# The end of an attention-and-two-MLPs kernel: turned row order in the last down parts, last sums in halves, one PSUM bank per output token row

## The chip, the cores and the metric

The kernel runs on one core of a Trainium2 chip. The metric is the device time of one execution in microseconds (us), as the median of several runs. Inputs and outputs are float32 in device memory.

## The reference

```python
def _attn_ref(x, weight_gen):            # x (2, 4096, 192), weight_gen (2, 4096, 8, 7)
    w = np.exp(weight_gen - np.max(weight_gen, axis=-1, keepdims=True))
    w = w / (np.sum(w, axis=-1, keepdims=True) + 1e-09)
    x_pad = np.concatenate([np.zeros((B, 6, D)), x], axis=1)
    x_unf = x_pad[:, np.arange(S)[:, None] + np.arange(7)[None, :], :].reshape(B, S, 7, 8, 24)
    return np.einsum('bshk,bskhg->bshg', w, x_unf).reshape(B, S, D)

def _moe_ref(x, w_in, w_out):            # w_in (192, 2048), w_out (2048, 192)
    h = x @ w_in
    return np.maximum(0.01 * h, h) @ w_out

def _moe2_ref(x, w_in, w_out):
    h = x @ w_in
    return np.where(h > 0.0, h, np.exp(np.minimum(h, 0.0)) - 1.0) @ w_out
```

The result is the second MLP of the first MLP of the attention's output, for 8192 tokens of 192 features.

## The kernel before, in words

**Tiling.** The 8192 tokens are cut into 16 chunks (CH) of 512 tokens (T): 128 partitions by 4 token rows (J). GpSimd and VectorE mix the seven taps of a chunk; then the chunk is turned so that features lie on partitions, and each MLP works on it in that form. The 192 features are carried as 128 ("a") and 64 ("b"). Products are made in split precision: a float32 operand is rounded into a "hi" part and a "lo" part, and hi times hi, lo times hi and hi times lo are added up in PSUM.

**Phases and steps.** A phase is one MLP on one chunk; there are 32 (0 to LAST = 31). Each has 8 steps (ST), numbered through as g = 0 to 255 (END). A step has an up part, which fills the 1024 columns of one half of the PSUM tensor `hidden`, an activation (ScalarE, VectorE), the rounding to `hid_hi` and the rest `hid_lo` (VectorE), and a down part of 20 matmuls, called by its step number d, which adds to the PSUM banks `y_a` (128 output features, 12 matmuls, helper `down_a`, L652) and `y_b` (64 features of the hi and the lo weights side by side on 128 partitions, 8 matmuls, helper `down_b`, L640). The down part of step d stands in TensorE's program beside the up part of step d + 3 (LAG). So the last three, d = 253, 254 and 255, have no up part beside them: they are the lone down parts (`down_alone` twice, `down_last` once).

**Row halves.** Every down matmul reads only 64 of the 128 rows of the hidden activations, LOW (partitions 0 to 63) or HIGH (64 to 127). A LOW and a HIGH matmul run side by side in the array, so 20 matmuls take ten places. Two matmuls of different halves that add to the same bank are kept apart by semaphores. In `y_b` all LOW matmuls of a part come first, then, behind a wait for `s_yblow`, all HIGH ones; the next part starts with LOW again, behind a wait for `s_dn`, which the part before raises with its last HIGH matmul. From d = 252 (APART) on `y_a` is summed apart, LOW in one bank and HIGH in the other, so that only `y_b` needs waits.

```python
                if d:
                    pe.wait_ge(s_dn, d)
                down_b(m, s, d, LOW, 0, 0)
```

**The last step.** Step 255 is made in halves of 512 columns on ScalarE and VectorE, and `down_last` waits for the first half of `hid_lo` (`s_lo1`), then for the second (`s_lo`).

**After the last matmul.** ScalarE copies one half of `y_a` into `ya` as soon as its matmuls are done (`s_yalast`, L925), and after the last matmul the 64 upper partitions of `y_b` into `ylow` (L919). VectorE then adds `yb` = `y_b` + `ylow` (L1129) and `ya` = `y_a` + `ya` (L1134), both for 512 columns. TensorE waits for both and turns the sums back to tokens (`transpose_last`): for each of the four token rows a 128x128 transpose of `ya` (L785) and a 64x64 one of `yb` (L786), two token rows to a bank of `hidden`. ScalarE copies the first two rows to `staged` (L940), VectorE the other two (L1251), and SyncE stores each half of `staged` with a DMA of its own (L499) when its copy is done. The end of the program waits for these DMAs.

Each engine runs its own program in the order written; the order is written out by hand in the functions below.

## Time and profile before

| | |
|---|---|
| median of 3 runs | 1143.02 us (1142.68 to 1144.25) |
| the profiled execution, its time | 1143.43 us |
| its span, first to last instruction | 1141.4 us |
| mean granted TensorE clock | 0.996 |
| TensorE matmul busy | 1126.3 us, 99% of the span |
| ScalarE, VectorE, GpSimd busy | 741.3 us (65%), 628.0 us (55%), 392.1 us (34%) |
| chain that ended last, share of TensorE | 97% |

TensorE is busy nearly the whole span; the rows used below come from its last 17 us, and a few from its first 60 us where the same kinds of instruction run. A matmul's row gives its start and a modelled length, and two rows of different halves can have the same start. "Before" in the notes in square brackets at a row's end is idle time of the engine and what ended it.

### The profile page before, as it was taken

The numbers are of one execution on the slowest core, as the hardware profiler recorded it, in microseconds if no ns is written. First come the engines' busy times: TensorE is split into PE (matmuls) and PEld (weight loads), VectorE is DVE, ScalarE is ACT, GpSimd is POOL, SyncE is SP. The second block draws the span as 40 slices with busy tenths as digits, with TensorE's granted clock in tenths as the row PEclk, the third lists the DMA queues.
The fourth block names the chain that finished last, engine by engine and source line by source line (L and its number), as shares of the span: only waits on it lengthen the run. The fifth ranks groups of instructions, "written<-read, shape, count | busy, mean of one in ns | idle before, by whom it ended". The sixth has DMA issues, their size and how long they took to land.

```text
span 1141.4 us, 22701 instructions
## 1 busy us (share of the span) xinstructions
PE 1126.3 (99%) x9804; PEld 923.7 (81%) x9804; DVE 628.0 (55%) x659; ACT 741.3 (65%) x830; POOL 392.1 (34%) x409
## 2 busy tenths in 40 slices
PE   6999999999999999999999999999999999999998
PEld 4778888888888888888888888888888888888886
DVE  7857737456464554636456464554736546364554
ACT  3666757567575765757667576665757667575774
POOL 5835340805317071350804308062260804400000
PEclk9999999999999999999999999999999999999999
DMA  5313021020202102021020211202021020110001
GB/s 178 107 63 95 1 81 29 29 82 1 90 20 69 41 29 81 1 81 29 29 81 1 81 29 44 67 15 84 12 81 29 29 81 2 43 29 29 15 1 56
DMA packets 44723, 55.45 MB, mean 49 GB/s; under 512 B 4116, under 2 KB 32914, under 8 KB 44624
## 3 DMA queue, kind: packets, MB, share of 16 engines
q1 hardware_dynamic: 44624, 54.01, 15.4%
q8 instruction: 77, 1.26, 0.5%
q14 instruction: 22, 0.18, 0.1%
HBM read 36.29 MB, written 17.69 MB: 47 GB/s over the span
## 4 chain that ended last, share of the span: by engine, by line
PE 97%; POOL 1%; DVE 1%; ACT 1%; DMA 1%; issue 0%; SPq 0%; POOLq 0%; ACTq 0%
PE y_a L652 31%; PE hidden L553 30%; PE y_b L640 20%; PE hidden L557 10%; PE hidden L608 5%; DMA xw<-in_x_dram 1%; DVE hid_lo L1178 0%; POOL prod L345 0%; ACT hid_hi L967 0%; POOL act L348 0%; POOL staged L345 0%; POOL act L345 0%; PE hidden L609 0%; PE hidden L785 0%; DVE dn L377 0%
## 5 line engine op out<-in xcount | busy, mean ns | idle before, releaser
L652 PE MATMUL y_a<-hid_hi,dn 64*128 64x512 f32 x2048 | 626.9, 386 | 0.1
L652 PEld LDWEIGHTS y_a<-hid_hi,dn 64*128 64x128 f32 x2048 | 375.8, 184 | 40.9 <-PE y_a L652 1.0
L640 PE MATMUL y_b<-hid_hi,dn 64*128 64x512 f32 x1024 | 396.1, 387 | 0.5 <-PE y_b L640 0.2
L640 PE MATMUL y_b<-hid_lo,dn 64*128 64x512 f32 x1024 | 395.4, 386 | 0.0
L652 PE MATMUL y_a<-hid_lo,dn 64*128 64x512 f32 x1024 | 394.6, 386 | 0.0
L1178 DVE TENSOR_TENSOR hid_lo<-hidden,hid_hi 128x1024 fp32r<-128x1024 f32 x128 | 156.5, 1223 | 256.8 <-ACT hid_hi L967 256.6
L553 PE MATMUL hidden<-in_a_hi,up_a_hi 64*128 64x512 f32 x1020 | 295.5, 388 | 2.2 <-DVE hid_lo L1178 1.7
L553 PE MATMUL hidden<-in_a_lo,up_a_hi 64*128 64x512 f32 x1020 | 294.7, 386 | 0.0
L553 PE MATMUL hidden<-in_a_hi,up_a_lo 64*128 64x512 f32 x1020 | 294.7, 386 | 0.0
L557 PE MATMUL hidden<-in_b,up_b_hi 64*128 64x512 f32 x1020 | 294.7, 386 | 0.0
L1178 DVE TENSOR_TENSOR hid_lo<-act,hid_hi 128x1024 fp32r<-128x1024 f32 x127 | 158.9, 1251 | 190.3 <-ACT hid_hi L967 190.3
L949 ACT ACTIVATE hidden<-hidden 128x1024 f32<-128x1024 f32 x127 | 128.0, 1008 | 199.3 <-PE hidden L557 199.3
L951 ACT ACTIVATE act<-hidden 128x1024 f32<-128x1024 f32 x127 | 130.5, 1027 | 160.9 <-PE hidden L557 159.1
L321 POOL TENSOR_TENSOR mix<-xw,wk 128x384 f32<-128x384 f32 x30 | 26.4, 880 | 573.9 <-DVE wk L1097 568.5
L640 PEld LDWEIGHTS y_b<-hid_hi,dn 64*128 64x128 f32 x1024 | 188.4, 184 | 21.9 <-issue 2.0
L652 PEld LDWEIGHTS y_a<-hid_lo,dn 64*128 64x128 f32 x1024 | 188.4, 184 | 20.0
L640 PEld LDWEIGHTS y_b<-hid_lo,dn 64*128 64x128 f32 x1024 | 188.4, 184 | 19.8
L333 POOL TENSOR_TENSOR mix<-mix,prod 128x384 f32<-128x384 f32 x180 | 191.9, 1066 | 2.4
L1153 DVE SCALAR_TENSOR_TENSOR act<-act,hidden 128x1024 f32<-128x1024 f32 x129 | 155.7, 1207 | 45.6 <-ACT act L956 45.1
L321 POOL TENSOR_TENSOR prod<-xw,wk 128x384 f32<-128x384 f32 x180 | 169.5, 949 | 9.4
L553 PEld LDWEIGHTS hidden<-in_a_hi,up_a_hi 64*128 64x128 f32 x1020 | 140.9, 184 | 25.3 <-issue 2.1
L553 PEld LDWEIGHTS hidden<-in_a_lo,up_a_hi 64*128 64x128 f32 x1020 | 141.0, 184 | 20.0
(109 smaller groups left out, 1318.8 us busy)
## 6 DMA issues: line engine op xcount, KB each, us to landing
xw<-in_x_dram SPq DMA_DIRECT2D x14, 960.0 KB
raw_b<-squares_out SPq DMA_DIRECT2D x60, 96.0 KB, 2.2
out_dram<-staged SPq DMA_DIRECT2D x15, 384.0 KB, 2.6
squares_in<-prod SPq DMA_DIRECT2D x56, 96.0 KB, 2.0
squares_out<-ya SPq DMA_DIRECT2D x15, 256.0 KB, 2.0
raw_a<-squares_in SPq DMA_DIRECT2D x14, 256.0 KB, 2.9
raw_d<-in_moe_w_out_dram SPq DMA_DIRECT2D x8, 384.0 KB, 3.4
raw_a<-in_moe_w_in_dram SPq DMA_DIRECT2D x8, 256.0 KB, 3.5
```

What stands on the lines that cost most here:

```text
L321: ops.tensor_tensor(dst, src, w, ALU.mult).then_inc(done, 1)
L333: ops.tensor_tensor(mix[:, j0:j1, :], mix[:, j0:j1, :], terms[k % n][:, j0:j1, :], ALU.add).then_inc(done, 1)
L553: return nc.tensor.matmul(hidden[:, s % 2, HALF[i]], w[m][rows, cols], v[src][rows, :], start=start, stop=stop)
L557: return nc.tensor.matmul(hidden[:, s % 2, HALF[i]], up_b_hi[m][rows, cols], in_b[src][rows, :], start=False, stop=stop)
L608: low = nc.tensor.matmul(hidden[:, s % 2, HALF[0]], up_b_lo[m][LOW, cols], in_b[src][LOW, :], start=False, stop=stop)
L640: return nc.tensor.matmul(y_b[d // ST % 2][:, :], dn[m][rows, f, P:2 * P], v[rows, s % HB, HALF[i]], start=start, stop=stop)
L652: return nc.tensor.matmul(y_a[bank][:, :], dn[m][rows, f, w:w + P], v[rows, s % HB, HALF[i]], start=start, stop=stop)
L949: nc.scalar.activation(hidden[:, s % 2, :], hidden[:, s % 2, :], ACT.Prelu, alpha=SLOPE).then_inc(s_leak, 1)
L951: nc.scalar.activation(act[:, s % 2, :], hidden[:, s % 2, :], ACT.Relu, scale=-1.0).then_inc(s_relu, 1)
L1153: nc.vector.scalar_tensor_tensor(out=a, in0=a, scalar=-1.0, in1=h, op0=ALU.add, op1=ALU.max).then_inc(done, 1)
L1178: nc.vector.tensor_tensor(hid_lo[:, s % HB, :], (act if m else hidden)[:, s % 2, :], hid_hi[:, s % HB, :].bitcast(f32), ALU.subtract).then ...
```

## The change

Three things are changed, all behind the last up part.

1. **The lone down parts.** Part 253 (new function `down_reversed`) and part 255 (`down_last`, rewritten) run the row halves the other way round: `y_b` HIGH first, then behind a wait LOW; part 254 stays as it was. So 252 ends with `y_b` HIGH and 253 begins with it, 253 ends with LOW and 254 begins with it, and so on; the wait for `s_dn` in front of 253, 254 and 255 is gone. `s_yblow` is called `s_ybfirst`. The half of `y_a` that is ready early is now LOW. `down_last` waits for the second half of `hid_lo` behind its fifth matmul, not its sixth.
2. **The last sums.** New function `add_last`: VectorE waits for the last matmul itself, adds `ya` first, in two halves of 256 columns (two token rows each), then `yb` in two halves. It no longer waits for `ylow` ahead of `ya`.
3. **The transposes.** Each token row goes to a bank of its own. Order: `ya` rows 0 and 1, `yb` rows 0 and 1, `ya` rows 2 and 3, `yb` rows 2 and 3, each group behind a wait for its half of the sum. ScalarE copies rows 0 and 2 to `staged`, VectorE rows 1 and 3; each of the two last stores waits for both engines.

TensorE's program, part 254's end and part 255 up to the sixth matmul, before (the name in front of the arrow is the PSUM bank written; L640 is `down_b`, L652 `down_a`):

```order
L652 MATMUL y_a0<-hid_lo,dn1 128x512
L640 MATMUL y_b1<-hid_lo,dn1 128x512
L640 MATMUL y_b1<-hid_hi,dn1 128x512 [waits down_done,half_hidden_lo_ready]
L652 MATMUL y_a1<-hid_hi,dn1 128x512
L640 MATMUL y_b1<-hid_lo,dn1 128x512
L652 MATMUL y_a1<-hid_hi,dn1 128x512
L652 MATMUL y_a0<-hid_hi,dn1 128x512
L652 MATMUL y_a1<-hid_lo,dn1 128x512
L640 MATMUL y_b1<-hid_hi,dn1 128x512 [waits hidden_lo_ready]
```

and the same place now (L642 is `down_b`, L654 `down_a`):

```order
L654 MATMUL y_a0<-hid_lo,dn1 128x512
L642 MATMUL y_b1<-hid_lo,dn1 128x512
L654 MATMUL y_a0<-hid_hi,dn1 128x512 [waits half_hidden_lo_ready]
L642 MATMUL y_b1<-hid_hi,dn1 128x512
L654 MATMUL y_a0<-hid_hi,dn1 128x512
L642 MATMUL y_b1<-hid_lo,dn1 128x512
L654 MATMUL y_a0<-hid_lo,dn1 128x512
L642 MATMUL y_b1<-hid_hi,dn1 128x512 [waits hidden_lo_ready]
L654 MATMUL y_a0<-hid_hi,dn1 128x512
```

The wait for the part before (down_done) is gone, and the wait for the second half of `hid_lo` has moved one matmul forward.

TensorE's transposes, before:

```order
L785 MATMUL hidden<-ident,ya 128x128 [waits y_b_added,y_a_copied]
L786 MATMUL hidden<-ident,yb1 128x64
L785 MATMUL hidden<-ident,ya 128x128
L786 MATMUL hidden<-ident,yb1 128x64
L785 MATMUL hidden<-ident,ya 128x128
L786 MATMUL hidden<-ident,yb1 128x64
L785 MATMUL hidden<-ident,ya 128x128
L786 MATMUL hidden<-ident,yb1 128x64
```

and now:

```order
L810 MATMUL hidden<-ident,ya 128x128 [waits y_a_copied]
L810 MATMUL hidden<-ident,ya 128x128
L813 MATMUL hidden<-ident,yb1 128x64 [waits y_b_added]
L813 MATMUL hidden<-ident,yb1 128x64
L810 MATMUL hidden<-ident,ya 128x128 [waits y_a_copied]
L810 MATMUL hidden<-ident,ya 128x128
L813 MATMUL hidden<-ident,yb1 128x64 [waits y_b_added]
L813 MATMUL hidden<-ident,yb1 128x64
```

The eight transposes are the same; they stand in pairs of one kind, with four waits in place of one.

VectorE's last four instructions before the end, before (L1129, L1134 and L1251 and the one ahead):

```order
L1167 TENSOR_TENSOR hid_lo<-act,hid_hi 128x512 [waits hidden_hi_ready]
L1129 TENSOR_TENSOR yb1<-y_b1,ylow 64x4x4x32 [waits squares_out_written,y_low_copied]
L1134 TENSOR_TENSOR ya<-y_a0,ya 128x4x4x32 [waits y_a_high_rows_copied]
L1251 COPY staged<-hidden 128x384 [waits out_stored,out_transposed]
L68 UNCONDITIONAL_BRANCH
```

and now:

```order
L1208 TENSOR_TENSOR hid_lo<-act,hid_hi 128x512 [waits hidden_hi_ready]
L1170 TENSOR_TENSOR ya<-y_a1,ya 128x4x2x32 [waits y_a_high_rows_copied,down_done]
L1170 TENSOR_TENSOR ya<-y_a1,ya 128x4x2x32
L1175 TENSOR_TENSOR yb1<-y_b1,ylow 64x4x2x32 [waits squares_out_written,y_low_copied]
L1175 TENSOR_TENSOR yb1<-y_b1,ylow 64x4x2x32
L1293 COPY staged<-hidden 128x192 [waits out_transposed,out_stored]
L1293 COPY staged<-hidden 128x192 [waits out_transposed]
```

Two adds have become four and one copy has become two; ScalarE's one copy (L940) has become two of 192 columns as well (L973).

The diff, cut to its core:

```diff
-        out_turn = hidden[:, 0, :]
+        out_bank = [hidden[:, j // 2, j % 2 * T:j % 2 * T + D] for j in range(J)]
...
+        BEHIND_REVERSED = (END - 1,)
...
-            for i, done, count in ((0, s_stag, CH), (1, s_stagv, 1)):
-                sp.wait_ge(done, count)
+            for i in (0, 1):
+                sp.wait_ge(s_stag, CH + i)
+                sp.wait_ge(s_stagv, 1 + i)
...
-                if d:
+                if d and d not in BEHIND_REVERSED:
...
+            def down_reversed(m, s, d):
+                pe.wait_ge(s_lo, d + 1)
+                down_a(m, s, d, LOW, 0, 0)
+                down_b(m, s, d, HIGH, 0, 0)
+                down_a(m, s, d, LOW, 0, 1)
+                down_b(m, s, d, HIGH, 0, 1)
+                down_a(m, s, d, LOW, 0, 2)
+                down_b(m, s, d, HIGH, 1, 0)
+                down_a(m, s, d, LOW, 1, 0)
+                down_b(m, s, d, HIGH, 1, 1).then_inc(s_ybfirst, 1)
+                if d < ST:
+                    pe.wait_ge(s_dn, d)
+                down_a(m, s, d, LOW, 1, 1)
+                down_a(m, s, d, HIGH, 0, 0)
+                down_a(m, s, d, LOW, 1, 2)
+                down_a(m, s, d, HIGH, 0, 1)
+                pe.wait_ge(s_ybfirst, d + 1)
+                down_b(m, s, d, LOW, 0, 0)
+                down_a(m, s, d, HIGH, 0, 2)
+                down_b(m, s, d, LOW, 0, 1)
+                down_a(m, s, d, HIGH, 1, 0)
+                down_b(m, s, d, LOW, 1, 0)
+                down_a(m, s, d, HIGH, 1, 1)
+                down_b(m, s, d, LOW, 1, 1)
+                down_a(m, s, d, HIGH, 1, 2).then_inc(s_dn, 1)
...
             def transpose_last():
...
+                for h in (0, 1):
+                    pe.wait_ge(s_ya, CH + h)
+                    turn_a(2 * h)
+                    turn_a(2 * h + 1)
+                    pe.wait_ge(s_yb, LAST + 1 + h)
+                    turn_b(2 * h)
+                    turn_b(2 * h + 1)
...
-            for d in range(LAG - 1, 0, -1):
-                down_alone(1, ST - 1 - d, END - d)
+            down_reversed(1, ST - 3, END - 2)
+            down_alone(1, ST - 2, END - 1)
             down_last()
...
-                nc.scalar.activation(staged[:, 0, :], out_turn[:, 0:2 * D], ACT.Copy).then_inc(s_stag, 1)
+                for j in (0, 2):
+                    act_e.wait_ge(s_outt, j + 1)
+                    nc.scalar.activation(staged[:, j // 2, 0:D], out_bank[j], ACT.Copy).then_inc(s_stag, 1)
...
+            def add_last():
+                dve.wait_ge(s_dn, END + 1)
+                dve.wait_ge(s_ya1, 1)
+                a, a0 = last_columns(ya[:, :], True), last_columns(y_a[LAST % 2][:, :], False)
+                b, b0, b1 = last_columns(yb[1][:, :], True), last_columns(y_b[LAST % 2][0:D2, :], False), last_columns(ylow[:, :], False)
+                halves = slice(0, J // 2), slice(J // 2, J)
+                for js in halves:
+                    nc.vector.tensor_tensor(a[:, :, js], a0[:, :, js], a[:, :, js], ALU.add).then_inc(s_ya, 1)
+                dve.wait_ge(s_ylow, LAST + 1)
+                dve.wait_ge(s_outw, 32 * (CH - 1))
+                for js in halves:
+                    nc.vector.tensor_tensor(b[:, :, js], b0[:, :, js], b1[:, :, js], ALU.add).then_inc(s_yb, 1)
...
-            nc.vector.tensor_copy(staged[:, 1, :], out_turn[:, T:T + 2 * D]).then_inc(s_stagv, 1)
+            for j in (1, 3):
+                dve.wait_ge(s_outt, j + 1)
+                nc.vector.tensor_copy(staged[:, j // 2, D:2 * D], out_bank[j]).then_inc(s_stagv, 1)
```

## Rows read from the trace of the kernel before

**Rows 1.** The page: the chain that ended last, by engine.

```profile
PE 97%; POOL 1%; DVE 1%; ACT 1%; DMA 1%; issue 0%; SPq 0%; POOLq 0%; ACTq 0%
```

**Rows 2.** The timeline of TensorE: start us, length us, instruction; parts 252 and 253.

```profile
1124.92 0.39 PE L640 MATMUL y_b<-hid_hi,dn 64*128 64x512 f32 x1
1125.14 0.39 PE L640 MATMUL y_b<-hid_lo,dn 64*128 64x512 f32 x1
1125.68 0.47 PE L640 MATMUL y_b<-hid_hi,dn 64*128 64x512 f32 x1 [0.15 <-PE y_b L640]
1125.99 0.39 PE L640 MATMUL y_b<-hid_lo,dn 64*128 64x512 f32 x1
1126.22 0.39 PE L640 MATMUL y_b<-hid_hi,dn 64*128 64x512 f32 x1
...
1126.45 0.39 PE L640 MATMUL y_b<-hid_lo,dn 64*128 64x512 f32 x1
...
1127.18 0.39 PE L640 MATMUL y_b<-hid_hi,dn 64*128 64x512 f32 x1
...
1127.40 0.39 PE L640 MATMUL y_b<-hid_lo,dn 64*128 64x512 f32 x1
...
1127.86 0.39 PE L640 MATMUL y_b<-hid_lo,dn 64*128 64x512 f32 x1
```

**Rows 3.** The same view, parts 254 (first row) and 255.

```profile
1128.39 0.46 PE L640 MATMUL y_b<-hid_hi,dn 64*128 64x512 f32 x1
...
1131.12 0.47 PE L640 MATMUL y_b<-hid_hi,dn 64*128 64x512 f32 x1
...
1132.12 0.39 PE L640 MATMUL y_b<-hid_lo,dn 64*128 64x512 f32 x1
...
1132.60 0.47 PE L640 MATMUL y_b<-hid_hi,dn 64*128 64x512 f32 x1
...
1133.37 0.39 PE L640 MATMUL y_b<-hid_lo,dn 64*128 64x512 f32 x1
```

**Rows 4.** The timeline of VectorE: `hid_lo` of step 254, then of step 255 in halves.

```profile
1125.85 1.23 DVE L1178 TENSOR_TENSOR hid_lo<-act,hid_hi 128x1024 fp32r<-128x1024 f32 x1 [0.24 <-ACT hid_hi L967]
...
1128.75 1.47 DVE L1167 TENSOR_TENSOR hid_lo<-act,hid_hi 128x512 fp32r<-128x512 f32 x2
```

**Rows 5.** The timeline of all engines behind the last matmul.

```profile
1133.80 0.59 ACT L919 ACTIVATE ylow<-y_b 64x512 f32<-64x512 f32 x1 [0.41 <-PE y_b L640]
1134.43 0.68 DVE L1129 TENSOR_TENSOR yb<-y_b,ylow 64x512 f32<-64x512 f32 x1 [4.21 <-ACT ylow L919]
1135.04 0.67 DVE L1134 TENSOR_TENSOR ya<-y_a,ya 128x512 f32<-128x512 f32 x1
...
1135.76 0.35 PE L785 MATMUL hidden<-ident,ya 128*128 128x128 f32 x1 [2.00 <-DVE ya L1134]
...
1136.04 0.37 PE L786 MATMUL hidden<-ident,yb 64*128 64x64 f32 x1
...
1136.34 0.47 PE L785 MATMUL hidden<-ident,ya 128*128 128x128 f32 x1
...
1136.74 0.37 PE L786 MATMUL hidden<-ident,yb 64*128 64x64 f32 x1
...
1138.14 0.37 PE L786 MATMUL hidden<-ident,yb 64*128 64x64 f32 x1
1138.55 0.56 DVE L1251 COPY staged<-hidden 128x384 f32<-128x384 f32 x1 [2.84 <-PE hidden L786]
1139.13 0.33 SPq L499 DMA_DIRECT2D out_dram<-staged  x1
```

**Rows 6.** Busy time by stretch; the third number from the end is the granted clock.

```profile
1135.50:1135.70 0.20, 0.00 (x0) 0.00 (x0) 0.20 (x1) 0.00 (x0) 0.00 (x0) 1.00 0.00 0
1135.90:1136.00 0.10, 0.10 (x1) 0.00 (x0) 0.00 (x0) 0.00 (x0) 0.00 (x0) 0.69 0.00 0
1136.00:1136.10 0.10, 0.10 (x2) 0.06 (x1) 0.00 (x0) 0.00 (x0) 0.00 (x0) 0.50 0.00 0
```

**Rows 7.** The timeline near the start: 128x128 products at the lower and the higher clock, and a reader.

```profile
9.28 1.87 PE L760 MATMUL y_b<-ident,prod 128*128 128x128 f32 x8 [2.78 <-POOL prod L345]
...
19.54 1.09 PE L764 MATMUL y_a<-ident,act 128*64 128x128 f32 x8
...
20.67 0.59 ACT L891 ACTIVATE in_b_up<-y_a 64x512 fp32r<-64x512 f32 x1 [0.42 <-PE y_a L764]
```

**Rows 8.** The timeline at 52 us: VectorE on 256 columns, and its next start.

```profile
52.37 0.41 DVE L376 TENSOR_TENSOR dn<-raw_d,dn 128x256 fp32r<-128x256 f32 x1
...
52.70 0.69 DVE L377 TENSOR_TENSOR dn<-raw_d,dn 128x512 fp32r<-128x512 f32 x1
```

More of the change, by code:

```diff
@@ L638, in down_b @@
                 v = (hid_hi, hid_lo)[n]
-                start, stop = f == 0 and n == 0 and rows == LOW, f == FT - 1 and n == 1 and rows == HIGH
+                start, stop = f == 0 and n == 0 and rows == LOW, f == FT - 1 and n == 1 and rows == (LOW if d == END else HIGH)
                 return nc.tensor.matmul(y_b[d // ST % 2][:, :], dn[m][rows, f, P:2 * P], v[rows, s % HB, HALF[i]], start=start, stop=stop)
@@ L672, in down_open @@
                 down_a(m, s, d, HIGH, 0, 2)
-                down_b(m, s, d, LOW, 1, 1).then_inc(s_yblow, 1)
+                down_b(m, s, d, LOW, 1, 1).then_inc(s_ybfirst, 1)
                 down_a(m, s, d, HIGH, 1, 0)
@@ L720, in down_last @@
                 wait_half_end(pe, s_lo, s_lo1, 0)
[L721 removed]
+                down_a(1, s, d, LOW, 0, 0)
+                down_b(1, s, d, HIGH, 0, 0)
+                down_a(1, s, d, LOW, 0, 1)
+                down_b(1, s, d, HIGH, 0, 1)
+                down_a(1, s, d, LOW, 0, 2)
+                wait_half_end(pe, s_lo, s_lo1, 1)
+                down_b(1, s, d, HIGH, 1, 0)
+                down_a(1, s, d, LOW, 1, 0)
+                down_b(1, s, d, HIGH, 1, 1).then_inc(s_ybfirst, 1)
+                down_a(1, s, d, LOW, 1, 1)
+                down_a(1, s, d, HIGH, 0, 0)
+                down_a(1, s, d, LOW, 1, 2).then_inc(s_yalast, 1)
+                down_a(1, s, d, HIGH, 0, 1)
+                pe.wait_ge(s_ybfirst, END + 1)
                 down_b(1, s, d, LOW, 0, 0)
[L723 removed]
+                down_a(1, s, d, HIGH, 0, 2)
                 down_b(1, s, d, LOW, 0, 1)
[L725 to L729 removed]
+                down_a(1, s, d, HIGH, 1, 0)
                 down_b(1, s, d, LOW, 1, 0)
[L731 to L732 removed]
                 down_a(1, s, d, HIGH, 1, 1)
[L734 to L745 removed]
+                down_b(1, s, d, LOW, 1, 1)
+                down_a(1, s, d, HIGH, 1, 2).then_inc(s_dn, 1)
             def sum_first_mix():
@@ L778, in transpose_last, with turn_a, turn_b @@
             def transpose_last():
-                pe.wait_ge(s_ya, CH)
-                pe.wait_ge(s_yb, LAST + 1)
-                for j in range(J):
-                    o = (j % 2) * D
-                    o += (j // 2) * T
-                    nc.tensor.transpose(out_turn[:, o:o + P], ya[:, j * P:(j + 1) * P], ident[:, :])
-                    last = nc.tensor.transpose(out_turn[:, o + P:o + D], yb[1][:, j * P:(j + 1) * P], ident[0:D2, 0:D2])
-                    if j % 2:
-                        last.then_inc(s_outt, 1)
+                def turn_a(j):
+                    nc.tensor.transpose(out_bank[j][:, 0:P], ya[:, j * P:(j + 1) * P], ident[:, :])
+                def turn_b(j):
+                    nc.tensor.transpose(out_bank[j][:, P:D], yb[1][:, j * P:(j + 1) * P], ident[0:D2, 0:D2]).then_inc(s_outt, 1)
+                for h in (0, 1):
[5 more added lines that the diff above has]
+                    turn_b(2 * h + 1)
             def phase(m, c, ph, dm, dc):
@@ L924, in take_y @@
                     act_e.wait_ge(s_outw, 32 * dc)
[L925 removed]
+                    nc.scalar.activation(last_columns(ya[:, :], True), last_columns(y_a[1 - ph % 2][:, :], False), ACT.Copy).then_inc(s_ya1, 1)
                     copy_low()
@@ L1126, in add_y @@
                 dst, b0, b1 = yb[dm][:, :], y_b[ph % 2][0:D2, :], ylow[:, :]
-                if ph == LAST:
-                    dst, b0, b1 = last_columns(dst, True), last_columns(b0, False), last_columns(b1, False)
                 nc.vector.tensor_tensor(dst, b0, b1, ALU.add).then_inc(s_yb, 1)
-                if ph == LAST:
-                    dve.wait_ge(s_ya1, 1)
-                    whole = last_columns(ya[:, :], True)
-                    nc.vector.tensor_tensor(whole, last_columns(y_a[1 - ph % 2][:, :], False), whole, ALU.add).then_inc(s_ya, 1)
+            def add_last():
[10 more added lines that the diff above has]
+                    nc.vector.tensor_tensor(b[:, :, js], b0[:, :, js], b1[:, :, js], ALU.add).then_inc(s_yb, 1)
             def turn_mix(c):
```

28 lines of the change are left out of this document (3 added, 25 removed).

## The prediction

> **What bounds the kernel now.** I read the page's chain first: 97% of the chain that ended last is TensorE [rows 1]. So a microsecond counts only where TensorE stands still or where nothing of it is left, and the change touches nothing ahead of the last up part. I therefore read only the last 17 us: the timeline of TensorE over the lone down parts, VectorE's timeline over the same stretch, then all engines behind the last matmul.
>
> The reader is to see three things. First, in steady state the pairs of a down part start 0.227 us apart, but between part 252 and 253 they start at 1125.14, 1125.68, 1125.99 and 1126.22 [rows 2]: three places take 1.08 us in place of 0.68, so the wait for the part before costs 0.40. The same gap, 0.53 and 0.54 from start to start, stands ahead of 254 (1127.86 to 1128.39) and of 255 [rows 2, 3]. Second, inside part 255 the last LOW matmul of `y_b` starts at 1132.12 and the first HIGH one at 1132.60 with a long first row, 0.47 [rows 3]: there too the drain shows. Third, from the start of the last matmul, 1133.37, to the issue of the last store, 1139.13, 5.76 us pass in single file: 0.43 to ScalarE's copy, its 0.59, two adds of 0.68 and 0.67 that start 0.61 apart, eight transposes from 1135.76 to 1138.14, a copy of 0.56 [rows 3, 5]. After the issue come 2.27 us to the span's end at 1141.4.
>
> **The lone parts.** The last pair of 252 starts at 1125.14 and the last of 255 at 1133.37: 8.23 us for 30 places. At 0.227 each they would take 6.81. All of the 1.42 goes if no wait is felt. Three boundaries are 1.20 of it, part 255's middle wait and small slips the rest. Do new waits take their place? The turned parts keep a wait in the middle, for the fourth `y_b` HIGH matmul, but now the first LOW one stands three places later, 0.68 us; a dependent matmul started 0.54 after its forerunner [rows 2], so it fits. Behind that wait stand all further matmuls of both halves, so if it did not fit, each part would pay up to the 0.40 of a boundary. `hid_lo` is the next thing that can be late. Part 254 would start at 1127.64 and its `hid_lo` ends at 1127.08; part 255 at 1129.91, its first half being ready near 1129.45. The second half is done at 1130.22 [rows 4], and TensorE now wants it ahead of the third pair, 1130.36, with the weight load in front of that. I charge 0.10 (bounds 0 and 0.40). ScalarE's and VectorE's work there does not wait for these down parts, so they get no earlier and no later. Gain 1.32; last pair at 1132.05.
>
> **The sums.** ScalarE's early copy of `y_a` starts 0.43 behind the sixth place of 255 and is done near 1132.1, ahead of need. VectorE can start 0.43 behind the last pair, at 1132.48. What half an add costs the tail does not show. Upper bound: as much as a whole one, 0.61 from start to start; lower: half of that. The nearest row has 256 columns: 0.41 long, the next starting 0.33 later [rows 8]. I take it. `ya` halves start at 1132.48 and 1132.81, `yb` halves at 1133.14 and 1133.47, ended at 1133.55 and 1133.88; `ylow` is ready at 1133.07 (0.59 behind 1132.48) and hides behind the `ya` adds. Were those faster, `ylow` would set the pace. Splitting is what a rule speaks against. The Trainium skill (Perfetto Trace Analysis, section "Optimizing Scalar/DVE Operations") gives VectorE an overhead of about 125 ns for each instruction that reads PSUM, and advises larger operations where the engine is saturated. As an estimate from that page the two extra adds cost 0.25, where the row's spacing implies 0.07 above 256 columns at the rate of the long rows, and the sum would be 0.1 worse by it.
>
> **The transposes.** A transpose starts 0.05 behind the add it waits for [rows 5]. Before, each change of kind costs a place of 0.40 (from `ya` to `yb`) or 0.30 (back), at a granted clock of 0.50; the first, mostly at full clock, took 0.28 [rows 5, 6]. Products of one kind in a row took 0.14 at the higher clock and 0.23 at the lower (1.09 and 1.87 for eight) [rows 7]. The granted clock fell from 1.00 to 0.50 (2.4 to 1.2 GHz) at about 1135.93, behind a stretch from 1133.76 in which TensorE did nothing but the first transpose [rows 6], 2.17 us after the last matmul ended. Now the standstill before the first transpose is 0.5 us, and all are through 2.4 us after the last matmul's end. I take the higher clock. First `ya` at 1132.94, second 1133.08; first `yb` at 1133.60 (1133.55 and 0.05), then 1133.74, `ya` 1134.02 and 1134.16, `yb` 1134.44 and 1134.58. A change of kind counts 0.28 (bounds 0.14 and 0.40). Its last row is 0.27 long (0.37, less 0.10 for the clock, as 0.47 became 0.35), and a reader starts 0.04 behind such a row (1138.51 to 1138.55; 20.63 to 20.67) [rows 5, 7]: 1134.89.
>
> **Copies and stores.** VectorE's copy of 384 columns took 0.56; 192 fewer at 1.09 ns, from 0.67 for 512 and 1.23 for 1024 [rows 4, 5], leave 0.35, bounds 0.28 and 0.56. It ends at 1135.24, the store is issued at 1135.26. ScalarE's row 2 copy runs beside. The first store now waits for both engines, but has both near 1134.4, and its issue is over before the second's; it costs nothing. If the two transfers met, the second would be later by at most its own 0.6 us of data. The bank of its own costs nothing: it lets two engines read while TensorE writes.
>
> **Sum.** From the last pair to the issue 3.21 us in place of 5.76: 2.55. With 1.32 the gain is 3.87: the profiled execution of 1143.43 would be 1139.56. It stands 0.41 above the median, which I keep: 1143.02 less 3.87 is **1139.2 us**. A measurement of this kernel can tell about 0.2%, 2.29 us, from no change; that bound is 1140.7.
>
> **Rivals.** (A) The clock falls before or during the new transposes. For: it did in the same place before. Against: the standstill is a quarter as long. Places of 0.23, 0.30 and 0.40 and a last row of 0.37 put the issue at 1135.77: gain 3.36, **1139.7**. The Trainium skill (TensorE: Matmul & The Clock Gate, section "Part 4: PE-mode transpose") says that transposes do not count as work for the clock; by that rule the eight would be part of the standstill and A likelier. The trace fits it as far as it goes: the clock fell while a transpose ran. (B) Halves cost as much as wholes. The last `yb` half ends at 1134.99 and the copy takes 0.56: gain 3.06, **1140.0**. For: short instructions near 0.4 us carry a large fixed part. Against: rows 8. (C) The drain in the middle of the two turned parts is felt, 0.40 each, so TensorE gains 0.52: gain 3.07, **1140.0**. Against: 0.68 is above 0.54, and in part 253 before, with the same distance, the wait cost nothing: 1126.45 to 1127.18 is three places and 0.05 [rows 2]. (D) A, B and C together: gain 2.07, **1141.0**, within 0.2%. (E) The other side: the turned parts lose their pairing. Their matmuls begin with `y_a` LOW beside `y_b` HIGH, an order that only the end of a part had. If each half waited for the other, 20 pairs would take 0.227 more each, 4.54: **1143.7**, slower than before; from 17 lost pairs on the gain is eaten, and on top of D it would be 1145.5. Against: the closing pairs of every part are just this mixture and run at 0.23 (1127.18, 1127.40) [rows 2].
>
> **How the numbers follow.** Forecast 0.50, A 0.20, B 0.08, C 0.10, D 0.08, E 0.04 (half of it within 0.2%, half slower). Faster by over 0.2%: 0.50 + 0.20 + 0.08 + 0.10 = 0.88. Within: 0.08 + 0.02 = 0.10. Slower: 0.02. Range: upward to D, 1141.1. Downward the cheap bounds: no wait for `hid_lo` (0.10), a change of kind at 0.14 (0.28), a copy of 0.28 (0.07), and some 0.3 by which runs of one kernel differ: 1138.4.
>
> **What would show it.** TensorE's last down pair should start near 1132.05 with no gap of 0.54 at 253, 254 and 255; VectorE's `ya` half some 0.43 behind it; spacing 0.33 of the adds; granted clock 1.00 through the transposes and the last of them near 1134.6; the last store issued near 1135.3. A gap at the seventh place of 253 or 255 would be C, a clock of 0.50 A, adds of 0.6 B, rows of one half alone E. If the span shrinks by less than 2 us though all this holds, the tail behind the last store has grown, and the sum misses it.

## The result and the profile after

The changed kernel took 1138.93 us, median of 7 runs (1138.55 to 1139.19), beside 1142.75 us for the kernel before on the same chip (median of 7, 1142.67 to 1144.25). The ratio is 0.9964, 95% interval 0.9953 to 0.9975: faster by 0.36%. Forecast: 1139.2, range 1138.4 to 1141.1.

| | before | after |
|---|---|---|
| the profiled execution, its time | 1143.43 us | 1139.19 us |
| its span | 1141.4 us | 1137.4 us |
| mean granted clock | 0.996 | 1.000 |
| TensorE matmul busy | 1126.3 us | 1125.1 us (99%) |
| ScalarE, VectorE, GpSimd busy | 741.3, 628.0, 392.1 us | 741.6, 628.4, 392.0 us |

The page of the changed kernel, the chain that ended last by engine, reads as [rows 1] did:

```profile
PE 97%; POOL 1%; DVE 1%; DMA 1%; ACT 0%; issue 0%; SPq 0%; POOLq 0%; ACTq 0%
```

TensorE's timeline in the changed kernel (start, length), the places that answer to [rows 2, 3]. L642 is now `down_b`, L654 `down_a`.

```profile
1125.22 0.39 PE L642 MATMUL y_b<-hid_lo,dn 64*128 64x512 f32 x1
...
1125.45 0.39 PE L642 MATMUL y_b<-hid_hi,dn 64*128 64x512 f32 x1
...
1126.13 0.39 PE L642 MATMUL y_b<-hid_lo,dn 64*128 64x512 f32 x1
...
1126.81 0.39 PE L642 MATMUL y_b<-hid_hi,dn 64*128 64x512 f32 x1
...
1127.49 0.39 PE L642 MATMUL y_b<-hid_lo,dn 64*128 64x512 f32 x1
...
1127.71 0.39 PE L642 MATMUL y_b<-hid_hi,dn 64*128 64x512 f32 x1
...
1130.44 0.42 PE L642 MATMUL y_b<-hid_hi,dn 64*128 64x512 f32 x1
...
1130.70 0.38 PE L642 MATMUL y_b<-hid_lo,dn 64*128 64x512 f32 x1
...
1132.08 0.39 PE L654 MATMUL y_a<-hid_lo,dn 64*128 64x512 f32 x1
```

The first two rows are the last pair of 252 and the first of 253: 0.23 apart, where 0.54 stood. From the fourth `y_b` HIGH (1126.13) to the first LOW (1126.81) it is 0.68, three places, and the LOW row has its normal length: the middle wait is not felt. 253 passes to 254 (1127.49, 1127.71) without a gap, and 254 to 255 too (1129.76, 1129.98, not shown). The row at 1130.44 is the one behind the wait for the second half of `hid_lo`, which was ready at 1130.31: 0.42 long, its follower 0.26 behind it, a slip of 0.03 to 0.04. From the last pair of 252 to the last of 255 it is 6.86 us (1125.22 to 1132.08), 8.23 before: 1.37 gained.

All engines behind the last matmul, answering to [rows 5]; "x2" is a group of two, whose length runs from the first's start to the second's end:

```profile
1131.54 0.60 ACT L958 ACTIVATE ya<-y_a 128x512 f32<-128x512 f32 x1 [1.96 <-PE y_a L654]
...
1132.50 0.59 ACT L952 ACTIVATE ylow<-y_b 64x512 f32<-64x512 f32 x1 [0.36 <-PE y_a L654]
1132.59 0.76 DVE L1170 TENSOR_TENSOR ya<-y_a,ya 128x256 f32<-128x256 f32 x2 [2.28 <-PE y_a L654]
...
1133.07 0.44 PE L810 MATMUL hidden<-ident,ya 128*128 128x128 f32 x2 [0.61 <-DVE ya L1170]
1133.26 0.74 DVE L1175 TENSOR_TENSOR yb<-y_b,ylow 64x256 f32<-64x256 f32 x2
...
1133.72 0.33 PE L813 MATMUL hidden<-ident,yb 64*128 64x64 f32 x2 [0.22 <-DVE yb L1175]
...
1133.99 0.44 PE L810 MATMUL hidden<-ident,ya 128*128 128x128 f32 x2
...
1134.36 0.33 PE L813 MATMUL hidden<-ident,yb 64*128 64x64 f32 x2
1134.60 0.90 SPq L501 DMA_DIRECT2D out_dram<-staged  x2
...
1134.73 0.36 DVE L1293 COPY staged<-hidden 128x192 f32<-128x192 f32 x1 [0.21 <-PE hidden L813]
```

Read it as two files of work that overlap. VectorE no longer waits for `ylow`: that copy and the `ya` adds start together. TensorE starts on the first half of `ya` while VectorE is on the next sum. From the start of the last down matmul to the end of VectorE's last copy it is 3.01 us (1132.08 to 1135.09), before 5.74 (1133.37 to 1139.11, [rows 3, 5]). Behind it 2.3 us remain to the span's end, as before.

Busy time by stretch (third number from the end: granted clock), over the last transposes and over the stores:

```profile
1134.20:1134.80 0.60, 0.49 (x4) 0.20 (x2) 0.39 (x2) 0.36 (x2) 0.00 (x0) 1.00 0.00 0
1135.00:1137.40 2.40, 0.00 (x0) 0.00 (x0) 0.09 (x1) 0.00 (x0) 0.00 (x0) 1.00 0.46 164
```

Where [rows 6] show the clock fall, here it stays at 1.00 to the end of the span, though TensorE does nothing in the second stretch. The account of the spans: 1.37 in the lone parts, 8.03 to 5.32 from the last down matmul's start to the span's end (2.71), less 0.08 by which part 252 ended later: 4.00.

### The profile page after: what moved, and what is told of

Read it like the earlier page. It is cut to its first block, busy times and chain, and to the rows that moved or that the text cites. A ratio compares the mean times of both kernels' runs of the same rounds, so it can differ in the third digit from the quotient of the medians.

```text
span 1137.4 us, 22704 instructions
## 1 busy us (share of the span) xinstructions
PE 1125.1 (99%) x9804; PEld 923.7 (81%) x9804; DVE 628.4 (55%) x662; ACT 741.6 (65%) x831; POOL 392.0 (34%) x409
## 4 chain that ended last, share of the span: by engine, by line
PE 97%; POOL 1%; DVE 1%; DMA 1%; ACT 0%; issue 0%; SPq 0%; POOLq 0%; ACTq 0%
PE y_a L654 31%; PE hidden L555 30%; PE y_b L642 20%; PE hidden L559 10%; PE hidden L610 5%; DMA xw<-in_x_dram 1%; DVE hid_lo L1219 0%; POOL prod L346 0%; ACT hid_hi L1000 0%; POOL act L349 0%; POOL staged L346 0%; POOL act L346 0%; PE hidden L611 0%; DVE dn L378 0%; PE y_b L789 0%
## 5 line engine op out<-in xcount | busy, mean ns | idle before, releaser
L654 PE MATMUL y_a<-hid_hi,dn 64*128 64x512 f32 x2048 | 626.6, 386 | 0.1
L654 PEld LDWEIGHTS y_a<-hid_hi,dn 64*128 64x128 f32 x2048 | 375.9, 184 | 41.0 <-PE y_a L654 1.0
L642 PE MATMUL y_b<-hid_hi,dn 64*128 64x512 f32 x1024 | 395.8, 386 | 0.0
L642 PE MATMUL y_b<-hid_lo,dn 64*128 64x512 f32 x1024 | 395.3, 386 | 0.0
L654 PE MATMUL y_a<-hid_lo,dn 64*128 64x512 f32 x1024 | 394.7, 386 | 0.0
L642 PEld LDWEIGHTS y_b<-hid_hi,dn 64*128 64x128 f32 x1024 | 188.4, 184 | 20.3 <-issue 0.4
L654 PEld LDWEIGHTS y_a<-hid_lo,dn 64*128 64x128 f32 x1024 | 188.4, 184 | 20.2
L642 PEld LDWEIGHTS y_b<-hid_lo,dn 64*128 64x128 f32 x1024 | 188.4, 184 | 20.0
L559 PEld LDWEIGHTS hidden<-in_b,up_b_hi 64*128 64x128 f32 x1020 | 141.0, 184 | 20.0
```

The costliest lines, as they stand in the source:

```text
L559: return nc.tensor.matmul(hidden[:, s % 2, HALF[i]], up_b_hi[m][rows, cols], in_b[src][rows, :], start=False, stop=stop)
L642: return nc.tensor.matmul(y_b[d // ST % 2][:, :], dn[m][rows, f, P:2 * P], v[rows, s % HB, HALF[i]], start=start, stop=stop)
L654: return nc.tensor.matmul(y_a[bank][:, :], dn[m][rows, f, w:w + P], v[rows, s % HB, HALF[i]], start=start, stop=stop)
```

## The experiments

Ratios are to the kernel before on the same chip, with the 95% interval. The variants ran on other chips than the first comparison; the kernel before took 1142.47, 1142.85 and 1142.90 us there (medians), so compare ratios, not times, across rows. One comparison is independent of the start of the run: from the last pair of part 252 (a `y_b` row of `hid_lo`) to that of 255 ("lone parts"), and from there to the end of VectorE's last copy ("tail"). It is needed because the first product of the mix (`ident`, `prod`, near the start) begins anywhere from 8.88 to 10.54 us in these profiles, and all behind it moves along.

| kernel | time, us | ratio | lone parts | tail | span |
|---|---|---|---|---|---|
| before | 1142.75 | | 8.23 | 5.74 | 1141.4 |
| before again | 1142.32 (one) | | 8.23 | 4.90 | 1140.2 |
| changed | 1138.93 | 0.9964 [0.9953, 0.9975] | 6.86 | 3.01 | 1137.4 |
| changed again | 1139.05 (one) | | 6.86 | 3.01 | 1137.3 |
| changed, parts as before | 1140.14 | 0.998 [0.9971, 0.9989] | 8.22 | 3.03 | 1139.8 |
| before, parts turned | 1141.4 | 0.999 [0.9981, 0.9999] | 6.86 | 5.70 | 1139.9 |
| whole sums | 1139.24 | 0.9971 [0.996, 0.9982] | 6.87 | 3.20 | 1137.3 |
| copies of two rows | 1139.11 | 0.9969 [0.9957, 0.998] | 6.85 | 3.29 | 1137.4 |
| kinds alternating | 1139.54 | 0.9972 [0.9961, 0.9983] | 6.86 | 3.70 | 1137.8 |
| sums interleaved | 1138.83 | 0.9963 [0.9951, 0.9976] | 6.86 | 2.96 | 1137.0 |
| and `ylow` in halves | 1138.57 | 0.9962 [0.9948, 0.9976] | 6.87 | 2.74 | 1136.8 |
| nearer waits | 1139.15 (one) | | 7.30 | 3.07 | 1137.4 |

Most steps between the changed kernel and its variants are smaller than the intervals; there the profile's rows decide, not the times.

### One half of the change alone

The changed kernel with the lone parts as before:

```diff
-            down_reversed(1, ST - 3, END - 2)
-            down_alone(1, ST - 2, END - 1)
+            for d in range(LAG - 1, 0, -1):
+                down_alone(1, ST - 1 - d, END - d)
...
-                if d and d not in BEHIND_REVERSED:
+                if d:
```

and `down_last` in its old order.

> The changed kernel with its sums, transposes and copies, but with the three lone down parts in the old order and the waits for the part before in place. My account (two separate gains): TensorE's last down pair starts 1.3 to 1.4 us later than in the changed kernel, with gaps of 0.54 us ahead of 253, 254 and 255, and everything behind it stands as it did; span near 1138.8, 2.6 us below the kernel before (1141.4). Rival (one gain only: the shorter sums would be covered by something else, or the turning carries it all): span within 0.5 us of 1141.4 or of 1137.4.

Its TensorE timeline, from the last pair of 252:

```profile
1126.24 0.39 PE L641 MATMUL y_b<-hid_lo,dn 64*128 64x512 f32 x1
...
1126.78 0.47 PE L641 MATMUL y_b<-hid_hi,dn 64*128 64x512 f32 x1 [0.15 <-PE y_b L641]
...
1128.96 0.39 PE L641 MATMUL y_b<-hid_lo,dn 64*128 64x512 f32 x1
...
1129.49 0.47 PE L641 MATMUL y_b<-hid_hi,dn 64*128 64x512 f32 x1
```

The gaps of 0.54 and 0.53 and the long first rows are back, the tail is 3.03. Its lone parts are 8.22 (1126.24 to 1134.46). The span of 1139.8 overstates the loss: the first mix product started at 10.54 (9.29 in the changed kernel) and part 252 ended 1.02 later. Without that the loss is 1.4.

The other half, only the lone parts turned, in the kernel before (the same functions, the tail untouched).

> The kernel before with nothing but the three lone down parts turned. My account: the last down pair starts near 1132.1, and the 5.76 us from it to the issue of the last store stay, transposes at a granted clock of 0.50; span near 1140.0, 1.4 below the kernel before. With e1 the gains should add up to the whole 4.0. Rival: with the matmuls closer the transposes keep the higher clock and the gain is 2 us or more; or it is lost behind the last matmul and the span stays at 1141.4.

Lone parts 6.86, tail 5.70, the granted clock again at 0.50 from the second transpose on. So by the rows the two halves of the change don't interact: 1.37 by the one, about 2.7 by the other, at these clocks. The medians say 1.07 and 2.33; their intervals (0.1 to 2.2 and 1.3 to 3.3) hold the rows' numbers but are too wide to check the sum.

### The sums

Whole adds of 512 columns, still `ya` first and each row in its bank:

```diff
-                halves = slice(0, J // 2), slice(J // 2, J)
+                halves = (slice(0, J),)
```

> The changed kernel with each of the two last sums added whole (512 columns), 128-feature sum still first, transposes in the same order. My account: first yb transpose 0.2 to 0.3 us later than 1.64 behind the last down pair, all behind it later by the same; span 0.2 to 0.3 longer than the changed kernel (1137.4). Rival (halves pay their fixed part twice and give nothing): span equal to the changed kernel or shorter.

VectorE's adds and the first transpose that waits for `yb`:

```profile
1132.21 0.69 DVE L1170 TENSOR_TENSOR ya<-y_a,ya 128x512 f32<-128x512 f32 x1 [2.29 <-PE y_a L654]
1132.82 0.67 DVE L1175 TENSOR_TENSOR yb<-y_b,ylow 64x512 f32<-64x512 f32 x1
...
1133.55 0.33 PE L813 MATMUL hidden<-ident,yb 64*128 64x64 f32 x2
```

It starts 1.83 behind the last pair (1131.72), 1.64 in the changed kernel, and all behind it is 0.19 later. As for what a half costs: two of `ya` take 0.76 where the whole takes 0.69. The Trainium skill (Perfetto Trace Analysis, section "Optimizing Scalar/DVE Operations") puts an instruction's overhead at about 125 ns; the extra one cost 0.07 here, and the split pays. The same section also advises to break up instructions of an engine that isn't saturated but holds up others, which is this case; the prediction named only its advice against splitting.

Sums in the order `ya`, `yb`, `ya`, `yb`:

```diff
                 for js in halves:
                     nc.vector.tensor_tensor(a[:, :, js], a0[:, :, js], a[:, :, js], ALU.add).then_inc(s_ya, 1)
-                dve.wait_ge(s_ylow, LAST + 1)
-                dve.wait_ge(s_outw, 32 * (CH - 1))
-                for js in halves:
+                    dve.wait_ge(s_ylow, LAST + 1)
+                    dve.wait_ge(s_outw, 32 * (CH - 1))
                     nc.vector.tensor_tensor(b[:, :, js], b0[:, :, js], b1[:, :, js], ALU.add).then_inc(s_yb, 1)
```

> The changed kernel with the four half sums in the order ya, yb, ya, yb. My account: ylow is ready 1.01 us behind the last down pair, the first yb half then ends 1.46 behind it in place of 1.59, the first yb transpose starts 0.12 earlier and so does all behind it; span 1137.3. Rival (the wait for ylow stands in front of the second ya half and pushes the last yb half back): the last yb transpose starts no earlier or up to 0.1 later, span 1137.4 or more.

The first `yb` transpose came 0.12 earlier (1.52 behind the last pair), as expected, but the end only 0.05: VectorE now waits for `ylow` inside the file of sums (its second instruction starts 0.55 behind the first, not 0.34), so the second half of `ya` ends at 1133.48 and the second pair of its transposes can start only at 1133.53, 0.33 behind the first pair of `yb` in place of 0.27. The wait for `ylow` showed what to try next, `ylow` copied in halves too:

```diff
-                    copy_low()
+                    for js in (slice(0, J // 2), slice(J // 2, J)):
+                        nc.scalar.activation(low[:, :, js], low0[:, :, js], ACT.Copy).then_inc(s_ylow, 1)
...
-                    dve.wait_ge(s_ylow, LAST + 1)
+                    dve.wait_ge(s_ylow, LAST + (1 if js.start == 0 else 2))
```

> The order of e7 (ya, yb, ya, yb halves) and ScalarE's copy of the upper partitions of y_b in two halves of 256 columns as well. My account: ylow's first half is ready 0.77 us behind the last down pair in place of 1.01, the four adds run without a gap from 0.50 on at a spacing of 0.33, the first yb half ends at 1.25 and the second at 1.91; first yb transpose at 1.30 (changed kernel 1.64, e7 1.52), second pair at 1.96 (changed 2.28, e7 2.22), last copy ends at 2.70 (changed 3.01). Median about 0.3 us below the changed kernel's. Rival (the copy's halves pay their fixed part twice and the second yb half waits for ylow's second half): second pair of yb transposes at 2.2 or later, no gain over e7.

```profile
1131.72 0.39 PE L654 MATMUL y_a<-hid_lo,dn 64*128 64x512 f32 x1
1132.14 0.65 ACT L963 ACTIVATE ylow<-y_b 64x256 f32<-64x256 f32 x2 [0.37 <-PE y_a L654]
1132.22 0.42 DVE L1174 TENSOR_TENSOR ya<-y_a,ya 128x256 f32<-128x256 f32 x1 [2.29 <-PE y_a L654]
1132.56 0.41 DVE L1177 TENSOR_TENSOR yb<-y_b,ylow 64x256 f32<-64x256 f32 x1
...
1133.07 0.34 PE L813 MATMUL hidden<-ident,yb 64*128 64x64 f32 x2
...
1133.72 0.33 PE L813 MATMUL hidden<-ident,yb 64*128 64x64 f32 x2
```

The four halves follow each other at 0.34 again, and the tail is 2.74 where 2.70 was expected. This version has the shortest tail and the lowest median, 0.36 below the changed kernel's but on another chip. The ratios (0.9962 and 0.9964) don't separate the two; the 0.27 of the profile's rows is what is shown.

### The order of the transposes

`ya`, `yb`, `ya`, `yb` row by row, as before the change, with banks and halves as after it:

```diff
                     turn_a(2 * h)
-                    turn_a(2 * h + 1)
                     pe.wait_ge(s_yb, LAST + 1 + h)
                     turn_b(2 * h)
+                    turn_a(2 * h + 1)
                     turn_b(2 * h + 1)
```

> The changed kernel with the transposes in the old alternating order (ya, yb, ya, yb of rows 0 and 1, then of 2 and 3), each in its own bank. My account: at the higher clock a change of kind costs about 0.13 more than a place of the same kind, and one ya transpose can no longer hide ahead of the first yb; the last transpose starts 0.6 to 0.8 us later than in the changed kernel (1134.49), span near 1138.1. Rival (a change of kind costs nothing at the higher clock): last transpose 0.15 later, span near 1137.6.

```profile
1133.39 0.27 PE L813 MATMUL hidden<-ident,yb 64*128 64x64 f32 x1 [0.33 <-DVE yb L1175]
...
1133.59 0.33 PE L810 MATMUL hidden<-ident,ya 128*128 128x128 f32 x1
...
1133.85 0.27 PE L813 MATMUL hidden<-ident,yb 64*128 64x64 f32 x1
...
1134.05 0.33 PE L810 MATMUL hidden<-ident,ya 128*128 128x128 f32 x1
```

At full clock a change of kind costs a place of 0.20 (from `yb` to `ya`) or 0.26 (back). In the changed kernel a pair of one kind ends 0.33 (`yb`) or 0.44 (`ya`) behind its start, that is 0.06 and 0.11 more than one transpose alone (0.27, 0.33). From the end of the first `yb` transpose to the end of the last it is six changes of kind and 1.38 us here, two changes and 0.70 in the changed kernel; the tail is 0.69 longer. One of the six transposes in that stretch is a `ya` that the changed kernel has already done while it waits for `yb`, so the 0.69 is the price of the order, not of the changes of kind alone. The span grew by 0.4 only, because part 252 ended 0.34 earlier than in the changed kernel's profile. This is the largest single piece that an experiment took out of the tail.

### The copies

Two token rows to a bank again, one copy of 384 columns by each engine, each store behind one engine. Pairing and halves stay:

```diff
-                for j in (0, 2):
-                    act_e.wait_ge(s_outt, j + 1)
-                    nc.scalar.activation(staged[:, j // 2, 0:D], out_bank[j], ACT.Copy).then_inc(s_stag, 1)
+                act_e.wait_ge(s_outt, 2)
+                nc.scalar.activation(staged[:, 0, :], hidden[:, 0, 0:2 * D], ACT.Copy).then_inc(s_stag, 1)
```

and the same on VectorE.

> The changed kernel with two token rows to a bank again and one copy of 384 columns on each engine, each store behind its own engine. My account: VectorE's last copy 0.56 in place of 0.36 us, so the last store is issued 0.2 later and the span is 0.2 longer (1137.6); the first store is issued about as early as before. Rival (the two stores meet, so the last one's end is set by the first): with the first store's start unchanged the span stays at 1137.4.

```profile
1134.10 0.34 PE L812 MATMUL hidden<-ident,yb 64*128 64x64 f32 x2
1134.55 0.56 DVE L1290 COPY staged<-hidden 128x384 f32<-128x384 f32 x1 [0.80 <-PE hidden L812]
```

The last copy takes 0.56 in place of 0.36, and starts 0.45 behind the transposes in place of 0.37: tail 3.29, 0.28 more. The span stayed at 1137.4, the rival's number, but only because part 252 ended 0.25 earlier in this profile. From the copy's end to the span's end it is 2.29, 2.31 in the changed kernel, so the two last stores do not get in each other's way in either form.

### The clock

Three copies of 768 columns, whose results nobody reads, ahead of VectorE's first sum, so that TensorE stands still as long as in the kernel before:

```diff
+                for spot in (raw_d[:, 4:8, :], mix[:, :, :], prod2[:, :, :]):
+                    nc.vector.tensor_copy(spot, raw_d[:, 0:4, :])
                 for js in halves:
```

> The changed kernel with three copies of 768 columns on VectorE ahead of the last sums, whose results nobody reads, so that TensorE stands still for some 2 to 3 us more before the transposes. Account A (the higher clock of the changed kernel's transposes comes from the short standstill): the granted clock falls to 0.50 before or during the transposes, and the stretch from the first yb transpose to the last goes from 0.77 to 1.1 us or more. Rival (the clock was kept for another reason, such as the order in pairs): clock 1.00 and the stretch stays at 0.77.

```profile
1133.99 0.44 PE L810 MATMUL hidden<-ident,ya 128*128 128x128 f32 x2 [2.00 <-DVE ya L1172]
...
1134.64 0.34 PE L813 MATMUL hidden<-ident,yb 64*128 64x64 f32 x2 [0.22 <-DVE yb L1177]
...
1135.28 0.33 PE L813 MATMUL hidden<-ident,yb 64*128 64x64 f32 x2
```

The stretches around the last pair (third number from the end: granted clock):

```profile
1135.20:1135.40 0.20, 0.20 (x4) 0.13 (x2) 0.20 (x1) 0.14 (x1) 0.00 (x0) 1.00 0.00 0
1135.40:1135.60 0.20, 0.20 (x2) 0.07 (x2) 0.04 (x1) 0.01 (x1) 0.00 (x0) 0.76 0.00 0
```

The idle time ahead of the first transpose is 2.00, exactly that of [rows 5], and still the transposes ran at 1.00, but for the last 0.1 us of the last pair; its pairs of `yb` start 0.64 apart, as in the changed kernel. The fall came 3.5 us behind the end of the last down matmul, not 2.17. Time 1140.12 (one run).

The kernel before, unchanged, once more.

> The kernel before once more, for the clock at its transposes and for the time at which its first products start. If the fall differs from run to run, it comes again somewhere between 2.2 and 4.9 us behind the last down matmul, so part or all of the transposes, which run from 2.0 to 4.7 us behind it, are at 0.50; a fall later than in the first profile would shorten the stretch of the transposes (2.38 us) by up to 0.9. From the last down pair of part 252 to the last of 255 8.2 us again.

```profile
1135.44 0.33 PE L785 MATMUL hidden<-ident,ya 128*128 128x128 f32 x1 [2.00 <-DVE ya L1134]
...
1137.09 0.27 PE L786 MATMUL hidden<-ident,yb 64*128 64x64 f32 x1
1137.39 0.56 DVE L1251 COPY staged<-hidden 128x384 f32<-128x384 f32 x1 [2.01 <-PE hidden L786]
```

```profile
1137.10:1137.40 0.30, 0.26 (x2) 0.12 (x1) 0.01 (x1) 0.00 (x0) 0.00 (x0) 1.00 0.00 0
```

The same program, all eight transposes at full clock: 1.65 us from the first start to the last in place of 2.38 [rows 5], tail 4.90 in place of 5.74. The clock's early fall is worth 0.84 us, and it happens in one execution of the kernel before and not in another.

Six such copies in place of three.

> e5 with six copies in place of three, so that TensorE stands still for about 3.4 us between the last down pair's end and the first transpose. Account now (the granted clock falls at a moment between 2.2 and more than 4.9 us behind the last down matmul that differs from run to run, as in the ten profiles so far): it falls before the last transpose, most or all of them run at 0.50, with about 1.1 us from the first yb transpose to the last in place of 0.70. Rival (transposes at this place keep the clock up however late they come): clock 1.00 to the last transpose.

TensorE stood still for 3.41 us, and only the last of the four pairs was slow (0.47 long in place of 0.33, clock 0.64 from 1137.10 to 1137.30). Time 1142.22 (one run); the fall came 4.6 us behind the last down matmul. That is later than expected: most or all of the transposes were to be slow.

The changed kernel once more.

> The changed kernel once more, for the same two things: last down pair of 252 to last of 255 6.9 us, from there to the end of VectorE's last copy 3.0, and the clock at 1.00 through the transposes, the last of which starts 2.3 to 2.4 us behind the last down pair. If the fall can come as early as in the kernel before (2.2 behind the last matmul's end), at most the last transpose would see it.

6.86 and 3.01 to the hundredth, the clock 1.00 through all transposes; it fell near 1134.87, 2.5 behind the last down matmul and 0.3 behind the last transpose. Over the 14 profiles the fall came at

| us behind the end of the last down matmul | profiles |
|---|---|
| 2.2, 2.3 | before; before with parts turned |
| 2.5, 2.7 | changed again; sums interleaved |
| 3.1, 3.3, 3.5, 3.6 | kinds alternating; copies of two rows; three extra copies; changed with parts as before |
| 4.0, 4.4, 4.6, 4.8 | whole sums; `ylow` in halves; six extra copies; before again |
| not within 4.9 | changed; nearer waits |

There is more order in this than the table shows. In the traces' record of the granted clock the last rise to 1.00, near the start, and the fall at the end lie 1123.0 us apart in eleven profiles and 1119.6 in the other three (changed again, before with parts turned, sums interleaved), each the same to 0.01. (In the changed kernel and the nearer waits the fall lies just behind the span's end, 5.0 and 5.1 behind the last down matmul.) The kernel before shows what that does: its last down matmul ended at 1133.77 and 1133.44 in its two profiles, but the clock had risen at 12.95 in the first and at 15.22 in the second, and it fell at 1135.94 and 1138.20. The rise came 2.27 us later, and so did the fall. So the moment of the fall goes with the moment of the rise, which differs between executions of one kernel; the length of TensorE's standstill alone does not give it. In the three profiles with the shorter stretch the last down matmul ended 1116.9 to 1117.3 behind the rise, in all others 1117.9 or more. No run moved the rise by itself, so that it causes the fall's moment isn't shown.

### The waits that did not show

`down_reversed` with its first `y_b` LOW one place (0.227 us) behind the last HIGH, and 254 with its first HIGH two places behind the last LOW (the order of the `y_a` matmuls changes to make room):

```diff
-                down_a(m, s, d, LOW, 1, 1)
-                down_a(m, s, d, HIGH, 0, 0)
-                down_a(m, s, d, LOW, 1, 2)
-                down_a(m, s, d, HIGH, 0, 1)
...
-            down_alone(1, ST - 2, END - 1)
+            down_nearer(1, ST - 2, END - 1)
```

> The changed kernel with the middle wait of part 253 one place behind the matmul that it waits for, and of part 254 two places behind it, in place of three. My account (a dependent matmul starts 0.54 behind its forerunner and the three places cover it): part 253 shows a gap of 0.54 between the two starts and costs about 0.40 more, part 254 a gap of about 0.48 to 0.54 and 0.1 to 0.2 more; last down pair 0.5 to 0.6 later than 1132.08 against the same stretch. Rival (the wait in the middle is never felt): both parts run at 0.227 a place and nothing is later.

```profile
1125.58 0.39 PE L642 MATMUL y_b<-hid_lo,dn 64*128 64x512 f32 x1
...
1126.03 0.49 PE L642 MATMUL y_b<-hid_hi,dn 64*128 64x512 f32 x1
...
1126.37 0.39 PE L642 MATMUL y_b<-hid_lo,dn 64*128 64x512 f32 x1
...
1128.21 0.39 PE L642 MATMUL y_b<-hid_lo,dn 64*128 64x512 f32 x1
...
1128.67 0.48 PE L642 MATMUL y_b<-hid_hi,dn 64*128 64x512 f32 x1
...
1129.00 0.38 PE L642 MATMUL y_b<-hid_lo,dn 64*128 64x512 f32 x1
```

The dependent matmul starts 0.45 to 0.46 behind its forerunner, and its own follower 0.33 to 0.34 behind it in place of 0.23. At one place's distance part 253 took 2.62 in place of 2.27, at two places part 254 took 2.40. At three, in the changed kernel, nothing. Together 0.44 more in the lone parts; the sum of the two is 0.48, but part 255 takes 2.06 from its first pair to its last in place of 2.10. It starts later here, `hid_lo` is ready in time, and the slip of 0.04 is gone.

## Why the prediction was right

**In total.** Forecast 1139.2, measured 1138.93. A gain of 3.87 was worked out; the medians of the comparison differ by 3.82, the spans by 4.00. That the total came so close owes something to luck: the sum was taken from a profile in which the clock had fallen early. From the second profile of the kernel before the same change is worth 3.26 (1.37 and 1.89), from the first 4.10, and the medians lie between the two.

**The lone parts** were right: 1.37 gained, 1.32 forecast; last pair at 1132.08, forecast 1132.05. The turned parts alone gave the 1.37, undoing them took it away, and there is no gap at any boundary. The term that was too large is `hid_lo`: charged 0.10, it cost 0.04, which the nearer waits gave back. Rival C was priced by the nearer waits: 0.35 at one place, 0.13 at two, none at three. So the reason given, that 0.68 is above the 0.54 of a dependent start, holds. But the distance at which nothing is felt is not the dependent start alone: at two places (0.45) that start was on time, at 0.46, and yet its follower came 0.11 late. Rival E did not occur: the turned pairs start 0.23 apart.

**The tail** was right in size, with terms that cancel. From the last pair to the end of VectorE's copy 3.19 was forecast, 3.01 measured. Two terms of the sum were mis-sized, in opposite directions:
- "VectorE can start 0.43 behind the last pair": it started 0.51 behind (0.49 to 0.52 in the other profiles, 0.57 with the nearer waits). ScalarE, on the same matmul, started 0.42 behind. The rows of before show only ScalarE in this place; its number was carried to another engine. Against the last pair the first `ya` transpose came 0.10 later than forecast and the first `yb` 0.09.
- "A change of kind counts 0.28": from start to start a change took 0.15 (from `yb` to `ya`) and 0.20 (back) behind a pair, 0.20 and 0.26 where the kinds alternate, and a second `yb` started 0.11 behind the first, a second `ya` 0.17, for which 0.14 was forecast. From the first `yb` transpose's start to the last's it took 0.75 (1133.72 to 1134.47), not 0.98. The 0.28 was taken from a place in which the clock was falling [rows 5, 6].
- The adds' spacing (0.33, measured 0.34) and the copy (0.35, measured 0.36) held. Rival B fell with them. (By its own rows, 0.33 less 256 columns at 1.09 ns, a half carries 0.05 extra, not the 0.07 that the text has; measured were 0.07.)

**The step that failed is the reason given for the clock.** The text gave two: the standstill is a quarter as long, and all transposes are through 2.4 us after the last matmul's end. The first does not hold: the length of the standstill alone does not decide. With the standstill of before put back, the transposes still ran at 1.00; with one of 3.41 three pairs of four did; and the kernel before itself runs at full clock through them in another execution. The clock falls at a moment that differs from one execution to the next, from 2.2 to beyond 4.9 us behind the last down matmul, and that goes with the moment of its rise near the start. The second is what the runs support. Transposes of the kernel before ran from 2.0 to 4.7 behind that point in its first profile, so they are sometimes caught; those of the changed kernel run from 0.6 to 2.2, ahead of every fall seen but for a few hundredths, and neither of its two profiles shows one caught. Rival A got its chance of 0.20 from the wrong comparison, that of the standstills. The Trainium skill (TensorE: Matmul & The Clock Gate, section "Part 4: PE-mode transpose") says that transposes are no work for the clock. These runs neither show nor exclude it: there are transposes in every one of them, and the fall came early in some and late in others.

This also splits the gain. At equal clock the tail gains 1.89 (4.90 to 3.01). The experiments take out of it 0.69 for the pairing of kinds, 0.28 for the copies and 0.19 for the halves of the sums, each alone from the changed kernel. The rest, about 0.7 if the three simply add (their sum was not tested), goes with what no single run took back: `ya` summed first, beside the copy of `ylow` instead of behind it. The rows show 0.55 of it: VectorE's first add starts 1.06 behind the last pair before, 0.51 now. Up to 0.84 more is had where the clock would have fallen. What sets the moment of the rise, and whether the fall follows from it, stays open.

## What to carry to other kernels

When matmuls of two row halves add to one bank, let each part begin with the half with which the last one ended, and let the second half start three places behind the last matmul of the first inside a part: here the drain then cost nothing. In a tail that runs in single file, split a step only where the next engine can start on the first piece, put first the sum whose inputs are ready first (argued from the rows, not tested alone), and issue transposes of one shape together. Line profiles up on an event shortly ahead of the change when the gain is near 1 us: the start of these runs alone moved by more than that, and the clock in the tail by 0.84.

## What was not expected of the hardware

- The granted clock's fall stands at no fixed distance behind the last down matmul: 2.2 to over 4.9 us, for the same two kernels in different executions (2.2 and 4.8 before; 2.5 and beyond 4.9 after). From the clock's last rise it stands at one of two distances, 1123.0 us in eleven profiles and 1119.6 in three.
- VectorE starts 0.07 to 0.10 us later than ScalarE on the same matmul's end (1132.59 and 1132.50 in the changed kernel, 1132.22 and 1132.14 with `ylow` in halves; 0.14 with the nearer waits). Whether the engine or its own second wait makes the difference, no run tells.
- Counted from end to end at full clock, a 64x64 transpose adds 0.06 us behind one of its kind and 0.20 behind a 128x128 one; a 128x128 one adds 0.11 behind its kind and 0.26 behind a 64x64 one.
- Behind a wait for the other half's matmul it is not only the dependent matmul that can be late (0.45 behind its forerunner at the earliest here): at two places' distance it was on time (0.46), and yet its follower came 0.33 behind it in place of 0.23.
